# First tile of a fused attention and two-layer expert kernel: where TensorE's first value block, gate blocks and scores stand

## The chip, the core and the metric

The kernel runs on one core of one Trainium2 chip. The metric is the device time of one execution in microseconds (us), the median of the runs shown. Profiles come from one profiled execution. Engines: TensorE (PE), VectorE (DVE), ScalarE (ACT), GpSimd (POOL), and SyncE (SP), which issues transfers. The granted clock of TensorE is given in shares of its full speed: 1.00 is 2.4 GHz, 0.50 is 1.2 GHz.

## What is computed

Three stages in float32, each on 1152 rows (2 batches of 576 tokens) of 512 columns. Top-32 attention with 8 heads of 64, a gated feed-forward layer, and an expert layer with 8 experts. Cut to what matters:

```
scores = q @ k.T / sqrt(64)                       # per batch and head, 576 x 576
kth = 32nd largest of each row;  scores below kth are masked
x = softmax(scores) @ v                           # heads side by side: 1152 x 512
xn = x / sqrt(mean(x*x) + 1e-6) * rms_g
x = (silu(xn @ w_gate) * (xn @ w_val)) @ w_out    # 512 -> 1536 -> 512
e = argmax(x @ r_gate);  p = softmax(x @ r_gate)[e]
out = p * (relu(x @ w1[e]) @ w2[e])               # at most 288 rows to an expert
```

## The kernel before

**Tiles, pairs and slots.** The rows are cut into 9 tiles of 128, the heads into 4 pairs. One pair of heads of one tile is a unit of attention work; there are 36, g = 0 to 35. Every engine runs a loop over slots n. In slot n VectorE finds the top 32 of pair n (eight at a time: MAX8, L1279, L1293 and L1301, and MATCH_REPLACE, L1285 and L1297), while the other engines carry pair g = n - 1 on: GpSimd makes the bias from the thresholds (L1468, L1472), ScalarE the marks (L1003), GpSimd takes them off the scores (L1480), ScalarE makes the exponentials in place (L1013), TensorE turns them in three parts (L489 for each head of the pair, in the text "the first turn" and "the second turn", and L495 for the rest of both), ScalarE copies each part to `pt` (L868), TensorE multiplies with v (L505, "the values"), and ScalarE copies the result to `oT` (L868) at the start of the next slot. In slot n TensorE also makes the scores of pair n + 1 (L478), which ScalarE copies to `s_ring` (L868).

**The dense work.** Feed-forward work of a finished tile is laid between the attention steps. A slot has three places, ALPHA, BETA and GAMMA; tables at the head of the file say in which slot and place a piece falls, counted from the slot FIRST = 6 for tile 0. There are three gate blocks (G) and three value blocks (V) of 512 columns. For tile 0 gate block 0 falls into slot 5 BETA, value block 0 into 6 ALPHA, gate block 1 into 6 BETA, value block 1 into 7 ALPHA, gate block 2 into 7 BETA, value block 2 into 7 GAMMA. Gate blocks go to the PSUM bank `blk[1]`, value blocks to `blk[0]`. ScalarE takes tanh of a gate block (L886), VectorE finishes silu from it and the bank (L1213), ScalarE copies a value block to `xrow` (L896), and GpSimd multiplies the two into `hid` (L1417). TensorE turns `hid` (L463) and multiplies with w_out (L548).

**High and low parts.** Matrices of this layer are multiplied as the sum of three products, high x high, high x low and low x high. The weights are split in tile 0's time, in 12 pieces of two 128 x 512 copies: ScalarE makes the high part of a piece (L868, `w_parts<-w_loads`), in slots and places after the table HIGH; GpSimd subtracts it for the low part (L1409), after the table LOW. The normalized rows are split as well: ScalarE writes `x_hi` in four parts of 128 columns (L972), VectorE `x_lo` (L1221). For tile 0 the blocks behind gate block 0 run as three groups of four: L522 (high x high), L525 (low rows), L528 (low weights). Gate block 0, and all blocks of later tiles, run L535 and L536 in turn and then L539.

**The turn of the last pair.** Three pairs of a tile are turned back into rows in the slot before (L463). The fourth goes in slot 5, ALPHA: TensorE turns `oT` (L627), a filler of one matmul follows (L563, "the bridge"), ScalarE copies to `xrow` (`raw_last_pair`, which signals `col_copied`), GpSimd divides by the sum (L1421), and TensorE turns that back (L632). Then ScalarE makes the fourth part of `x_hi`.

**Order.** Each engine runs what stands in its program in that order, and waits at semaphores. On SyncE's queue the load of w_out and the rows of q for tile 2 are issued one behind the other (L369, L319). The rest of the kernel, from about 490 us, is the expert layer.

Of the kernel before, what the change touches and what calls it, by code (L numbers as in the profile page):

```python
# [34 lines left out]
FIRST = 6  # L35
# [13 lines left out]
X2, LOGITS, PICK, LEXP, RANK, SEND = 10, 11, 12, 14, 15, 16  # L49
LAST = 16  # L50
HIGH = {0: (0, GAMMA), 1: (0, GAMMA), 2: (0, GAMMA), 3: (0, GAMMA), 4: (1, GAMMA), 5: (1, GAMMA),
        6: (2, GAMMA), 7: (3, GAMMA), 8: (4, GAMMA), 9: (5, GAMMA), 10: (6, GAMMA), 11: (6, GAMMA)}
LOW = {0: (0, GAMMA), 1: (0, GAMMA), 2: (1, ALPHA), 3: (1, ALPHA), 4: (2, ALPHA), 5: (2, ALPHA),
       6: (3, ALPHA), 7: (4, ALPHA), 8: (5, ALPHA), 9: (6, ALPHA), 10: (7, ALPHA), 11: (7, BETA)}
HIGH_ORDER, LOW_ORDER = tuple(HIGH), tuple(LOW)
# [5 lines left out]
def build(nc, q, k, v, w_gate, w_val, w_out, rms_g, r_gate, w1, w2, out, capacity):  # L61
# [13 lines left out]
    NG = NT * HP  # L75
# [17 lines left out]
    with ctx:  # L93
# [146 lines left out]
        def due(n, at, k):  # L240

            t, off = divmod(n - FIRST - k // 3, HP)
            return t if k % 3 == at and off == 0 and 0 <= t < NT else None
# [176 lines left out]
        def _(pe):  # L420
# [139 lines left out]
            def bridge(count):  # L560

                for _ in range(count):
                    mm(blk[1][:, 0:384], ident[:], kT[0][:, 0, 0:384], start=True, stop=True)  # L563
# [54 lines left out]
            def turn_last_pair(n, t):  # L618


                for i in (3, 4):
                    before = due(n, ALPHA, OUT[i][0])
                    if before is not None:
                        ffn_out(before, i)
                    if i == 3:
                        pe.wait_ge(s["o_copied"], HP * (t + 1))
                        tr(last_ps, oT[:, HP - 1, :], ident[:]).then_inc(s["col_full"], 1)  # L627
                if t == 0:
                    bridge(1)
                pe.wait_ge(s["normed"], 2 * t + 2)  # L630
                pe.wait_ge(s["x_hi_set"], CD * t + CD - 1)
                tr(tb[:, (HP - 1) * P:HP * P], xrow[:, (HP - 1) * P:HP * P], ident[:]).then_inc(s["col_turned"], 1)  # L632

            def dense(n, at):


                for i in range(FB):
                    t = due(n, at, V[i])
                    if t is not None:
                        if i > 0:  # L640
                            pe.wait_ge(s["val_copied"], t * 3 + i)
                        elif t > 0:
                            pe.wait_ge(s["out_copied"], t)
                        ffn_block(t, (wv_hi, wv_lo), i, blk[0])
                t = due(n, at, HID[1])
                if t is not None:
                    turn_hidden(t, 1)
                for i in range(3):
                    t = due(n, at, OUT[i][0])
                    if t is not None:  # L650
                        if i == 0:
                            pe.wait_ge(s["wo_in"], 16)
                            pe.wait_ge(s["val_copied"], t * 3 + 3)
                        ffn_out(t, i)
                t = due(n, at, HID[2])
                if t is not None:
                    turn_hidden(t, 2)
                for i in range(FB):
                    t = due(n, at, G[i])
                    if t is not None:  # L660
                        if t * 3 + i > 0:
                            pe.wait_ge(s["silu_done"], t * 3 + i)
                        else:
                            pe.wait_ge(s["k1_copied"], KC)
                        ffn_block(t, (wg_hi, wg_lo), i, blk[1])
                t = due(n, at, LOGITS)
                if t is not None:

                    if t == NT - 1:
                        stay_awake(AWAKE[0])  # L670
                    pe.wait_ge(s["r_in"], 16)
                    pe.wait_ge(s["t_free"], use["lg", t])
                    for c in range(CD):
                        last = mm(tb[:, 0:E], dcol[:, c * P:(c + 1) * P], wr[:, c, :], start=(c == 0), stop=(c == CD - 1))
                    last.then_inc(s["t_full"], 1)
                    if t == NT - 1:
                        stay_awake(AWAKE[1])
                t = due(n, at, HID[0])
                if t is not None:
                    turn_hidden(t, 0)  # L680
                t = due(n, at, RANK)
                if t is not None:


                    pe.wait_ge(s["picked"], t + 1)
                    if t > 0:
                        pe.wait_ge(s["seen_set"], t)
                    pe.wait_ge(s["t_free"], use["rk", t])
                    mm(tb[:, 0:E], upper[:], onehot[:], start=True, stop=False)
                    mm(tb[:, 0:E], ones[:], seen[:], start=False, stop=True).then_inc(s["t_full"], 1)  # L690
# [8 lines left out]
            for n in range(SLOTS):  # L699
# [8 lines left out]
                if t is not None:  # L708
                    dense(n, ALPHA)
                    turn_last_pair(n, t)  # L710
                    if n + 1 < NG:
                        scores(n + 1)
                    dense(n, BETA)
                    if probs:
# [6 lines left out]
                else:  # L721
# [9 lines left out]
                    if 0 <= g < HP:  # L731
                        pe.wait_ge(s["k_acted"], KC - 1)
                        if g > 1:
                            pe.wait_ge(s["k1_copied"], min(2 * g - 2, KC))
                        bridge(EARLY[g > 0])
                    if probs:
                        turn_probs(g, 0)
                    if g == HP - 1:
# [2 lines left out]
                    for i in (2 * n - 4, 2 * n - 3):  # L741
                        if 0 <= i < KC:
# [3 lines left out]
                            if i >= 2:  # L746
                                pe.wait_ge(s["k1_copied"], i - 1)
                            turn_keys(1, i, blk[i % 2])
                    dense(n, BETA)
                    turn_out(n)  # L750
                    if probs:
                        turn_probs(g, 1)
# [437 lines left out]
        def _(dve):  # L1190
# [24 lines left out]
            def low_part(n, first=False):  # L1215
                t = due(n, ALPHA, XB)
                if t is not None and first == (t == 0):

                    dve.wait_ge(s["x_hi_set"], CD * (t + 1))
                    for c in range(CD):  # L1220
                        last = vec.scalar_tensor_tensor(out=x_lo[:, c * P:(c + 1) * P], in0=tb[:, c * P:(c + 1) * P], scalar=gain[:, c:c + 1],  # L1221
                                                        in1=x_hi[:, c * P:(c + 1) * P], op0=ALU.mult, op1=ALU.subtract)
                    last.then_inc(s["t_free"], 1)
# [40 lines left out]
            for n in range(SLOTS):  # L1264
# [15 lines left out]
                for a in range(2):  # L1280
# [4 lines left out]
                    vec.match_replace(w_top[:, a, :], m8[:, 2 * (n % 2) + a, 0, :], s_ring[:, n % SR, a, :], NEG).then_inc(s["top_step"], 1)  # L1285
                    if a == 0:
                        beside(n - 1, GAMMA)
                low_part(n, True)
                for i in (1, 2):
                    for a in range(2):  # L1290

                        dve.wait_ge(s["top_step"], done + 4 * i - 2 + a + 1)
                        vec.max(m8[:, 2 * (n % 2) + a, i, :], w_top[:, a, :]).then_inc(s["top_step"], 1)  # L1293
                    for a in range(2):

                        dve.wait_ge(s["top_step"], done + 4 * i + a + 1)
                        vec.match_replace(w_top[:, a, :], m8[:, 2 * (n % 2) + a, i, :], w_top[:, a, :], NEG).then_inc(s["top_step"], 1)  # L1297
                    beside(n, (ALPHA, BETA)[i - 1])
# [243 lines left out]
```

## Time and profile before

| | us |
|---|---|
| median of 3 runs | 658.88 (657.09 to 659.9) |
| the profiled execution | 659.04 |
| its span, first to last instruction | 657.2 |
| TensorE busy | 620.1 (94%), x3954 |
| VectorE busy | 411.8 (63%) |
| ScalarE busy | 327.2 (50%) |
| GpSimd busy | 264.3 (40%) |
| mean granted clock of TensorE | 0.987 |

Busy time counts overlapping parts of an engine once. Times inside the trace are counted from the start of the span. A row of a timeline may merge several instructions (x4); what stands in square brackets is the engine's idle time before it, and what ended that.

### The profile page before, as it was taken

To read this page: it belongs to the slowest core of one execution; us is meant where nothing else is said; L and a number is where in the kernel's file an instruction comes from. 1 tells how busy PE (TensorE), PEld (TensorE's weight loads), DVE (VectorE), ACT (ScalarE), POOL (GpSimd) and SP (SyncE) were. 2 spreads that over 40 slices of the span, in tenths; PEclk is the share of its full clock that TensorE was granted. 3 is DMA by queue.
4 is the path that set the end of the run, shared out by engine and by line. 5 is a ranking of instruction groups with operands and counts; after the bars stand their busy time and mean duration, and the time that the engine had idled before them with its cause. 6 is when DMAs were issued, how large, how long until landed. Compare 5 with 4: busy or idle time off the path is not lost.

```text
span 657.2 us, 11168 instructions
## 1 busy us (share of the span) xinstructions
PE 620.1 (94%) x3954; PEld 476.8 (73%) x3954; DVE 411.8 (63%) x912; ACT 327.2 (50%) x713; POOL 264.3 (40%) x366
## 2 busy tenths in 40 slices
PE   6789899999999999999999999999999999999994
PEld 5465665775775775765766766756669999999994
DVE  5999997898898897897997996921111111111110
ACT  5777766766756756756766766743210101111100
POOL 2866764555454364364454453552310100111101
PEclk9799899999999999999999999999999999999998
DMA  9999700000000000000000000000396767767501
GB/s 242 204 382 334 202 5 0 9 26 1 17 17 2 18 17 0 17 17 1 17 17 1 1 17 1 0 18 1 103 392 221 259 225 257 245 217 268 170 1 38
DMA packets 55182, 65.45 MB, mean 100 GB/s; under 512 B 32282, under 2 KB 32282, under 8 KB 55132
## 3 DMA queue, kind: packets, MB, share of 16 engines
q1 hardware_dynamic: 53388, 60.05, 28.8%
q0 software_dynamic: 1744, 4.76, 2.0%
q8 instruction: 28, 0.46, 0.3%
q14 instruction: 22, 0.18, 0.1%
HBM read 52.89 MB, written 12.30 MB: 99 GB/s over the span
## 4 chain that ended last, share of the span: by engine, by line
PE 80%; ACT 9%; POOL 6%; issue 3%; DMA 1%; SPq 0%; POOLq 0%; ACTq 0%
PE ps L809 11%; PE ps L795 11%; PE ps L548 11%; PE ps L535 7%; PE ps L539 7%; PE ps L536 7%; PE ps L505 5%; PE ps L478 5%; PE ps L489 4%; PE ps L463 3%; POOL s_ring L1480 3%; ACT pt L868 2%; PE ps L563 2%; POOL hid L1417 2%; ACT z_pair L1003 1%
## 5 line engine op out<-in xcount | busy, mean ns | idle before, releaser
L1480 POOL TENSOR_TENSOR s_ring<-s_ring,z_pair 128x576 f32<-128x576 f32 x72 | 101.0, 1425 | 71.1 <-ACT z_pair L1003 71.1
L1297 DVE MATCH_REPLACE8 w_top<-m,w_top 128x576 f32<-128x576 f32 x144 | 105.9, 744 | 0.0
L1293 DVE MAX8 m<-w_top 128x8 f32<-128x576 f32 x144 | 101.7, 748 | 0.0
L548 PE MATMUL ps<-wo_space,hid 128*128 128x512 f32 x216 | 99.3, 593 | 0.4 <-issue 0.4
L535 PE MATMUL ps<-w_parts,x_hi 128*128 128x512 f32 x196 | 81.8, 417 | 0.0
L536 PE MATMUL ps<-w_parts,x_hi 128*128 128x512 f32 x196 | 77.5, 395 | 0.0
L809 PE MATMUL ps<-arena,w_loads 128*128 128x168 f32 x512 | 75.8, 307 | 0.5 <-issue 0.5
L795 PE MATMUL ps<-arena,w_loads 128*128 128x168 f32 x512 | 74.3, 306 | 0.6 <-ACT arena L868 0.6
L1503 POOL DMA_INDIRECT out_rows<-arena,s_ring x16 | 15.1, 944 | 147.0 <-DVE arena L1321 144.6
L795 PEld LDWEIGHTS ps<-arena,w_loads 128*128 128x128 f32 x512 | 73.3, 190 | 0.9 <-ACT arena L868 0.9
L809 PEld LDWEIGHTS ps<-arena,w_loads 128*128 128x128 f32 x512 | 73.2, 190 | 0.6 <-issue 0.6
L1013 ACT ACTIVATE s_ring<-s_ring,nbias 128x576 f32<-128x576 f32 x72 | 55.8, 775 | 25.5 <-POOL s_ring L1480 25.5
L548 PEld LDWEIGHTS ps<-wo_space,hid 128*128 128x128 f32 x216 | 37.8, 190 | 34.5 <-issue 34.5
L1279 DVE MAX8 m<-s_ring 128x8 f32<-128x576 f32 x72 | 52.0, 750 | 14.2 <-ACT s_ring L868 14.2
L505 PE MATMUL ps<-pt,arena 128*64 128x128 f32 (+1 forms) x800 | 49.6, 274 | 7.1 <-ACT pt L868 7.1
L1003 ACT ACTIVATE z_pair<-s_ring,nbias 128x576 f32<-128x576 f32 x72 | 51.7, 769 | 8.9 <-POOL nbias L1468 8.9
L505 PEld LDWEIGHTS ps<-pt,arena 128*64 128x64 f32 x800 | 41.0, 141 | 19.5 <-issue 10.1
L489 PE MATMUL ps<-ident,s_ring 128*128 128x128 f32 x288 | 44.6, 277 | 9.8 <-ACT pt L868 5.5
L539 PE MATMUL ps<-w_parts,x_lo 128*128 128x512 f32 x196 | 53.7, 396 | 0.0
L1285 DVE MATCH_REPLACE8 w_top<-m,s_ring 128x576 f32<-128x576 f32 x72 | 53.3, 744 | 0.0
L868 ACT ACTIVATE pt<-ps 128x512 f32<-128x512 f32 (+1 forms) x108 | 48.9, 489 | 8.3 <-PE ps L489 8.3
L1301 DVE MAX8 m<-w_top 128x8 f32<-128x576 f32 x72 | 50.8, 748 | 0.0
(142 smaller groups left out, 887.0 us busy)
## 6 DMA issues: line engine op xcount, KB each, us to landing
w_loads<-in_moe_w SPq DMA_DIRECT2D x16, 2048.0 KB, 8.9
dispatched_rows<-drow SPq DMA_DIRECT2D x18, 260.0 KB, 8.1
w_loads<-in_moe_w_gate SPq DMA_DIRECT2D x3, 1024.0 KB, 7.2
w_loads<-in_moe_w_val SPq DMA_DIRECT2D x3, 1024.0 KB, 9.4
wo_space<-in_moe_w_out SPq DMA_DIRECT2D x1, 3072.0 KB, 12.1
arena<-dispatched_rows SPq DMA_DIRECT2D x8, 341.2 KB
out_rows<-drow SPq DMA_DIRECT2D x9, 256.0 KB, 4.9
q_space<-in_q SPq DMA_DIRECT2D x8, 256.0 KB, 3.0
```

Source lines behind the costliest of these rows:

```text
L489: last = tr(pt_ps[:, j * P:(j + 1) * P], s_ring[:, g % SR, a, a * KL + j * P:a * KL + (j + 1) * P], ident[:])
L505: last = mm(oT_ps[a * D:(a + 1) * D, r0:r1], vs[b][:, j, 2 * hp + a, :], pt[:, at + r0:at + r1], start=(j == 0), stop=(j == KC - 1))
L535: mm(bank, x_hi[:, c * P:(c + 1) * P], w_hi[:, c, :], start=(c == 0), stop=False)
L536: mm(bank, x_hi[:, c * P:(c + 1) * P], w_lo[:, c, :], start=False, stop=False)
L539: last = mm(bank, x_lo[:, c * P:(c + 1) * P], w_hi[:, c, :], start=False, stop=(c == CD - 1))
L548: last = mm(blk[0], hid[:, c * P:(c + 1) * P], wo_s[:, c, :], start=(c == 0), stop=(c == CF - 1))
L795: last = mm(ps[:, 2 + n % 2, (f % 2) * MAIN:(f % 2 + 1) * MAIN], w1_s[par][:, c, f * P:(f + 1) * P], xT[par][:, c, :], start=(c == 0), sto ...
L809: last = mm(ps[:, 4 + n, (d % 2) * MAIN:(d % 2 + 1) * MAIN], w2_s[par][:, f, d * P:(d + 1) * P], hT[:, f, :], start=(f == 0), stop=(f == C ...
L868: return nc.scalar.activation(dst, src, ACT.Copy)
L1293: vec.max(m8[:, 2 * (n % 2) + a, i, :], w_top[:, a, :]).then_inc(s["top_step"], 1)
L1297: vec.match_replace(w_top[:, a, :], m8[:, 2 * (n % 2) + a, i, :], w_top[:, a, :], NEG).then_inc(s["top_step"], 1)
L1480: gp.tensor_tensor(row, row, z_pair[:, a, :], ALU.subtract).then_inc(s["lowered"], 1)
```

## The change

Five edits, all on the first tile but for one comparison that leaves the later tiles as they are:

- TensorE: value block 0 of tile 0 runs right behind gate block 0 in slot 5 (BETA), no longer in slot 6 (ALPHA).
- TensorE: in slots 6 and 7 the work of BETA (gate blocks 1 and 2) stands ahead of both turns, no longer between them.
- TensorE: in slot 5 the scores of pair 6 stand between the bridge and the second turn of the last pair (behind a new wait for `col_copied`), no longer behind that turn.
- ScalarE: the high part of piece 8 moves from slot 4, GAMMA, to slot 5, ALPHA, between the marks and the exponentials.
- VectorE: `x_lo` of tile 0 moves behind the next two MAX8.

```diff
-        6: (2, GAMMA), 7: (3, GAMMA), 8: (4, GAMMA), 9: (5, GAMMA), 10: (6, GAMMA), 11: (6, GAMMA)}
+        6: (2, GAMMA), 7: (3, GAMMA), 8: (5, ALPHA), 9: (5, GAMMA), 10: (6, GAMMA), 11: (6, GAMMA)}
...
                 if t == 0:
                     bridge(1)
+                    pe.wait_ge(s["col_copied"], 1)
+                    scores(n + 1)
                 pe.wait_ge(s["normed"], 2 * t + 2)
...
                 for i in range(FB):
                     t = due(n, at, V[i])
-                    if t is not None:
+                    if t is not None and t + i > 0:
...
                         ffn_block(t, (wg_hi, wg_lo), i, blk[1])
+                        if t + i == 0:
+
+                            ffn_block(t, (wv_hi, wv_lo), i, blk[0])
...
                     turn_last_pair(n, t)
-                    if n + 1 < NG:
+                    if t > 0 and n + 1 < NG:
                         scores(n + 1)
...
                         bridge(EARLY[g > 0])
+                    early = n in (FIRST, FIRST + 1)
+                    if early:
+                        dense(n, BETA)
                     if probs:
                         turn_probs(g, 0)
...
-                    dense(n, BETA)
+                    if not early:
+                        dense(n, BETA)
                     turn_out(n)
...
-                low_part(n, True)
                 for i in (1, 2):
                     for a in range(2):
 
                         dve.wait_ge(s["top_step"], done + 4 * i - 2 + a + 1)
                         vec.max(m8[:, 2 * (n % 2) + a, i, :], w_top[:, a, :]).then_inc(s["top_step"], 1)
+                    if i == 1:
+                        low_part(n, True)
```

TensorE, slot 5, from the first turn of the last pair to the scores of pair 7. Before:

```order
L627 MATMUL ps<-ident,oT 128x128
L563 MATMUL ps<-arena,ident 128x384
L632 MATMUL ps<-ident,xrow 128x128
L478 MATMUL ps<-arena,q_cols 128x288 x4
...
L539 MATMUL ps<-w_parts,x_lo 128x512 x4
L489 MATMUL ps<-ident,s_ring 128x128 x8
L495 MATMUL ps<-ident,s_ring 128x128
L505 MATMUL ps<-pt,arena 64x128 x10
L522 MATMUL ps<-w_parts,x_hi 128x512 x4
L525 MATMUL ps<-w_parts,x_lo 128x512 x4
L528 MATMUL ps<-w_parts,x_hi 128x512 x4
L478 MATMUL ps<-arena,q_cols 128x288 x4
```

and now (L634 is the line that was L632):

```order
L627 MATMUL ps<-ident,oT 128x128
L563 MATMUL ps<-arena,ident 128x384
L478 MATMUL ps<-arena,q_cols 128x288 x4
L634 MATMUL ps<-ident,xrow 128x128
...
L539 MATMUL ps<-w_parts,x_lo 128x512 x4
L522 MATMUL ps<-w_parts,x_hi 128x512 x4
L525 MATMUL ps<-w_parts,x_lo 128x512 x4
L528 MATMUL ps<-w_parts,x_hi 128x512 x4
L489 MATMUL ps<-ident,s_ring 128x128 x8
L495 MATMUL ps<-ident,s_ring 128x128
L505 MATMUL ps<-pt,arena 64x128 x10
L478 MATMUL ps<-arena,q_cols 128x288 x4
```

The scores (L478) moved ahead of the last pair's second turn, and the three groups of value block 0 ahead of both turns of the probabilities (L489 x8 is both). The left-out rows are those of gate block 0.

TensorE, slot 6, from the scores of pair 7 to the values of pair 5. Before:

```order
L478 MATMUL ps<-arena,q_cols 128x288 x4
L463 MATMUL ps<-ident,q_space 128x128 x4
L489 MATMUL ps<-ident,s_ring 128x128 x4
L522 MATMUL ps<-w_parts,x_hi 128x512 x4
L525 MATMUL ps<-w_parts,x_lo 128x512 x4
L528 MATMUL ps<-w_parts,x_hi 128x512 x4
L489 MATMUL ps<-ident,s_ring 128x128 x4
L495 MATMUL ps<-ident,s_ring 128x128
L463 MATMUL ps<-ident,hid 128x128 x4
L505 MATMUL ps<-pt,arena 64x128 x10
```

and now:

```order
L478 MATMUL ps<-arena,q_cols 128x288 x4
L463 MATMUL ps<-ident,q_space 128x128 x4
L522 MATMUL ps<-w_parts,x_hi 128x512 x4
L525 MATMUL ps<-w_parts,x_lo 128x512 x4
L528 MATMUL ps<-w_parts,x_hi 128x512 x4
L489 MATMUL ps<-ident,s_ring 128x128 x8
L495 MATMUL ps<-ident,s_ring 128x128
L463 MATMUL ps<-ident,hid 128x128 x4
L505 MATMUL ps<-pt,arena 64x128 x10
```

Gate block 1 stood between the two turns and now stands ahead of both. In slot 7 gate block 2 moves in the same way.

ScalarE, end of slot 4 to the first exponential of slot 5. Before:

```order
L868 ACTIVATE arena<-ps 128x4x64
L868 ACTIVATE w_parts<-w_loads 128x512 x2
L868 ACTIVATE oT<-ps 128x128
L868 ACTIVATE xrow<-ps 128x128
L972 ACTIVATE x_hi<-ps,gain 128x128 x4
L977 ACTIVATE hid,ssq<-xrow 128x512
L1003 ACTIVATE z_pair<-s_ring,nbias 128x576 x2
L1013 ACTIVATE s_ring,den<-s_ring,nbias 128x576
```

and now (each line number is 9 higher):

```order
L877 ACTIVATE arena<-ps 128x4x64
L877 ACTIVATE oT<-ps 128x128
L877 ACTIVATE xrow<-ps 128x128
L981 ACTIVATE x_hi<-ps,gain 128x128 x4
L986 ACTIVATE hid,ssq<-xrow 128x512
L1012 ACTIVATE z_pair<-s_ring,nbias 128x576 x2
L877 ACTIVATE w_parts<-w_loads 128x512 x2
L1022 ACTIVATE s_ring,den<-s_ring,nbias 128x576
```

The two copies of piece 8 (`w_parts<-w_loads`) moved from ahead of the `oT` copy to behind the marks.

## Rows read from the trace of the kernel before

**Rows 1.** Windows of TensorE: stretch, length, busy us (instructions), granted clock, DMA share, GB/s.

```profile
60.00:98.00 38.00, 33.12 (x200) 0.96 0.49 130
115.00:450.00 335.00, 325.50 (x2078) 1.00 0.04 11
```

**Rows 2.** Timeline of TensorE, slot 5: start, us, engine, line, operation, count, idle before.

```profile
60.36 0.33 PE L627 MATMUL ps<-ident,oT 128*128 128x128 f32 x1 [0.56 <-ACT oT L868]
...
61.92 0.30 PE L632 MATMUL ps<-ident,xrow 128*128 128x128 f32 x1 [0.59 <-ACT x_hi L972]
62.15 1.24 PE L478 MATMUL ps<-arena,q_cols 64*128 64x288 f32 x8
63.32 0.50 PE L535 MATMUL ps<-w_parts,x_hi 128*128 128x512 f32 x1
...
66.38 0.66 PE L489 MATMUL ps<-ident,s_ring 128*128 128x128 f32 x4
68.89 0.63 PE L489 MATMUL ps<-ident,s_ring 128*128 128x128 f32 x4 [1.86 <-ACT pt L868]
...
70.37 2.24 PE L505 MATMUL ps<-pt,arena 128*64 128x128 f32 x20 [0.74 <-ACT pt L868]
72.54 1.85 PE L522 MATMUL ps<-w_parts,x_hi 128*128 128x512 f32 x4
...
76.19 1.24 PE L478 MATMUL ps<-arena,q_cols 64*128 64x288 f32 x8
```

**Rows 3.** Windows of TensorE again, shorter stretches with idle time in them.

```profile
12.00:16.00 4.00, 2.59 (x18) 1.00 1.13 349
...
43.00:48.00 5.00, 4.52 (x27) 1.00 1.06 382
...
70.50:71.00 0.50, 0.50 (x8) 0.59 1.31 237
```

**Rows 4.** Timeline of ScalarE, end of slot 4 to slot 6.

```profile
58.96 1.18 ACT L868 ACTIVATE w_parts<-w_loads 128x512 fp32r<-128x512 f32 x2
...
65.46 0.78 ACT L1013 ACTIVATE s_ring<-s_ring,nbias 128x576 f32<-128x576 f32 x1 [0.89 <-POOL s_ring L1480]
...
68.16 0.58 ACT L868 ACTIVATE pt<-ps 128x512 f32<-128x512 f32 x1
...
72.68 0.28 ACT L868 ACTIVATE oT<-ps 128x128 f32<-128x128 f32 x1 [0.74 <-PE ps L505]
...
76.29 0.69 ACT L896 ACTIVATE xrow<-ps,rinv 128x512 f32<-128x512 f32 x1 [0.25 <-PE ps L528]
77.50 0.65 ACT L868 ACTIVATE s_ring<-ps 128x576 f32<-128x576 f32 x1 [0.52 <-PE ps L478]
...
79.82 0.61 ACT L868 ACTIVATE pt<-ps 128x512 f32<-128x512 f32 x1
81.28 0.69 ACT L886 ACTIVATE hid<-ps,rinv 128x512 f32<-128x512 f32 x1 [0.86 <-PE ps L528]
```

**Rows 5.** Timeline of GpSimd, slot 7.

```profile
86.10 2.81 POOL L1480 TENSOR_TENSOR s_ring<-s_ring,z_pair 128x576 f32<-128x576 f32 x2 [4.60 <-ACT z_pair L1003]
```

**Rows 6.** Timeline of TensorE, slots 6 and 7.

```profile
78.21 1.18 PE L522 MATMUL ps<-w_parts,x_hi 128*128 128x512 f32 x4
...
81.08 0.60 PE L489 MATMUL ps<-ident,s_ring 128*128 128x128 f32 x4
...
82.68 1.31 PE L505 MATMUL ps<-pt,arena 128*64 128x128 f32 x20 [0.45 <-ACT pt L868]
...
94.92 1.20 PE L528 MATMUL ps<-w_parts,x_hi 128*128 128x512 f32 x4 [0.56 <-POOL w_parts L1409]
```

**Rows 7.** Timeline of VectorE, slot 5.

```profile
62.66 1.13 DVE L1221 SCALAR_TENSOR_TENSOR x_lo<-ps,gain,x_hi 128x128 fp32r<-128x128 f32 x4 [1.59 <-ACT x_hi L972]
```

**Rows 8.** SyncE's queue at 59.57, and the landing times of loads into q_space.

```profile
59.57 0.91 SPq L319 DMA_DIRECT2D q_space<-in_q  x1
...
DMA to landing us min/median/max: 2.8/3.0/12.9
```

More of the change, by code:

```diff
@@ L638, in dense @@
                     t = due(n, at, V[i])
-                    if t is not None:
+                    if t is not None and t + i > 0:
                         if i > 0:
                             pe.wait_ge(s["val_copied"], t * 3 + i)
-                        elif t > 0:
+                        else:
                             pe.wait_ge(s["out_copied"], t)
```

## Prediction, made before the changed kernel was run

> **What bounds the kernel now.** I read the windows by stage first. TensorE is busy 325.50 of 335.00 us between 115 and 450, but only 33.12 of 38.00 us between 60 and 98, at a mean granted clock of 0.96 [rows 1]. So the long middle is TensorE's own work in program order, and time can only be won where TensorE waits before it: slots 5 to 7, the first tile. Whatever TensorE is ahead by at the end of slot 7 should be kept to the end, since nothing after it is tied to a fixed time.
>
> In slot 5 [rows 2] the reader is to see three losses: 0.56 us before L627; 1.86 us between the two turns of the probabilities (L489), and 0.74 us before the values (L505); and then the clock. It is granted in full up to 70.5 and is then at half (1.2 GHz) [rows 3], so that L505 takes 2.24 us where it takes 1.31 in the next slot, and the L522 of the value block 1.85 against 1.18 [rows 2, 6]. In slot 7 TensorE waits once more, 0.56 us, for the low part of a weight piece from GpSimd (L1409), before the third group of value block 2, at 94.92 [rows 6]. That wait is the one that ends last in this stage: before it GpSimd is released only at 86.10, after 4.60 us of idle time for ScalarE's marks [rows 5].
>
> **Part 1, piece 8's high copies move from slot 4 to slot 5.** On ScalarE they stood before the copy to oT: 1.18 us for two, or 1.04 in a row with others [rows 4]. The 0.56 us that TensorE waited for oT go, and 0.1 of overlap with it: L627 at 59.71 instead of 60.36, 0.65 earlier. In slot 5 the copies stand between marks and exponentials, where ScalarE waited 0.89 us for GpSimd [rows 4]; the marks come 0.15 earlier, so 1.04 lies in a hole of 0.89 + 0.15. I price it at nothing; without that cover it costs 1.0 of ScalarE.
>
> **Part 2, scores ahead of the last pair's second turn.** They take 1.17 us (62.15 to 63.32), and fill the time in which TensorE waited 0.59 us for x_hi before L632 [rows 2]. From L627 to the gate block were 63.32 - 60.36 = 2.96; without the 0.59 and the bridge's small overlap it is 2.3, and 59.71 + 2.3 = 62.0: 1.3 us earlier, 0.65 of it from part 1. The added wait is for ScalarE's copy behind L627, which is done while the bridge runs; it costs nothing, and is bounded by the 0.59 that it replaces. Behind it on TensorE stands everything, so if that copy came late all would.
>
> **Part 3, VectorE.** It stood 1.59 us for x_hi before x_lo [rows 7]; now two MAX8 (1.3 us) come first. VectorE gains about 1.4, and x_lo is ready by 63.6, before the gate block's eight high matmuls end at 64.0. So nothing new waits. VectorE's gain is of no use here: its thresholds are ready before ScalarE and GpSimd take them up.
>
> **Part 4, value block 0 behind gate block 0.** Gate 3.06 us (63.32 to 66.38), value 2.87 at full clock (78.21 to 81.08) [rows 2, 6]: from 62.0 TensorE is busy to 67.95. The first turn follows at once, ends at 68.55 (0.6 long, as at 81.08 [rows 6]), and ScalarE copies it at 68.62 instead of 68.16 [rows 4]. From that copy to the second turn are 0.73 us and from there to the values 1.48 (68.16, 68.89, 70.37) [rows 2, 4], so the values start at 70.83, 0.46 late. Of 1.86 + 0.74 us of idle time 0.8 + 0.74 stay. I take the clock as full there: 1.25 for the values instead of 2.17 gives 72.08 against 72.54. ScalarE has its own copies in front until 72.32, so oT goes from 72.68 to 72.32, 0.36 us earlier. That is all that the critical chain has won by here, although scores of pair 7 on TensorE are now at 72.7 instead of 76.19 [rows 2]: TensorE has gained 3.5 us, of which nearly all is value block 0, taken out of its way.
>
> **Part 5, slot 6.** ScalarE's chain starts 0.36 earlier. On it lay two waits for TensorE, 0.25 us before the value copy and 0.52 before the score copy [rows 4]; both go, with 0.2 us of overlap lost at them. So the copy of the first turn, at 79.82 [rows 4], comes at 79.82 - 0.36 - 0.97 = 78.5. TensorE had the gate block between the turns; now it stands before them, from 74.4 (scores and the turn of q take 1.7 after 72.7) to 77.2, and TensorE idles from 77.8 to the second turn at 78.5 + 0.73 = 79.2. This 1.4 us is the wait that replaces the old ones. Behind the copy ScalarE waited 0.86 us for the gate block [rows 4]; that goes too, 0.2 to 0.3 of it comes back as a wait for the second turn. 1.33 + 0.86 - 0.2 = 2.0 us: the hidden copy, the four weight copies and oT of slot 7 come 2.0 earlier.
>
> One load is moved nearer to its use. The rows of q for tile 2 are issued at 59.57, and the longest landing of that tile is 12.9 us [rows 8]: 72.5. The turn is now at 73.9, a margin of 1.4; I price it at nothing. If it landed w later than 73.9, the idle time before the second turn would cover 0.7 of it.
>
> Gate block 1 now also stands earlier behind its wait for silu 0. That follows ScalarE's tanh right behind the copies of slot 5 and one operation of VectorE, so by about 72; the margin is 2 us, and gate block 2 has 3 or more in slot 7. I price both at nothing.
>
> **Part 6, slot 7.** Marks, and with them GpSimd's run from 86.10, come 2.0 earlier, at 84.1. GpSimd works without a pause from there to the low part of piece 11, so this ends at 92.9 instead of 94.9, and the third group of value block 2 starts there instead of at 94.92 [rows 5, 6]. TensorE by its own path: values at 80.67, value block 1 and scores to 86.1, gate block 2 to 88.96, second turn 90.35 after a hole of 0.9 (0.73 behind the copy again), value block 2 from 90.9, its third group two thirds of 2.87 behind, at 92.9. The two paths meet within 0.1, so **both must be early for the gain to be 2.0 us**.
>
> **Sum.** 0.36 + 0.97 + 0.66 = 2.0. Profiled execution: 659.04 - 2.0 = 657.0; its span 657.2 becomes 655.2. The median of the runs shown, 658.88, stands 0.16 under it, which gives 656.9. The bounds: below, if every wait in slots 5 to 7 went and the clock stayed full, 0.56 + 0.59 + 1.86 + 0.74 + 0.56 and 0.93 + 0.67 of clock, 5.9 us; above, the rival on the clock.
>
> **Rival 1, the clock falls in slot 6.** The half clock in slot 5 came after idle times of 1.86 and 0.74 us close together. In the stretch 12 to 16, with 2.59 us busy of 4 and one idle time of 1.4 us, it did not fall [rows 3]. My new hole in slot 6 is 1.4 us with 0.3 more behind it, nearer to the second row. If it falls, L505 and L522 pay 0.93 + 0.67 = 1.6 us on TensorE's path, which has no slack: gain 0.4, 658.5. The page "TensorE: Matmul & The Clock Gate" of the Trainium skill says ("HAM oscillation") that idle gaps over about 3 us are to be avoided; by it neither hole would count, but the trace disagrees, for the longest idle time before the fall here was 1.86.
>
> **Rival 2, the clock falls in slot 5 all the same.** After 67.95 come only turns, with holes of 0.8 and 0.74, until 70.8. The values then take 0.93 more, oT comes at 73.2, and ScalarE's chain with it: 2.0 - 0.9 = 1.1 gained, 657.8. Against it: in 43 to 48, which holds the same kind of turns around one hole of 0.74, the clock stayed at 1.00 [rows 3]. The same page of the Trainium skill (Part 4, PE-mode transpose) says that transposes do not count as busy like matmuls; by that rule this rival is the likely one. The row at 43 to 48 leans against it, but bridges stand in that stretch too.
>
> **Rival 3, more than the sum.** If ScalarE's copies fit the holes better than I place them, TensorE could keep more of the 3.5 us that it is ahead by at 72.7. GpSimd's run from 86.10 speaks against it. It would give 3.5 to 4.5: 654.9.
>
> **Rival 4, slower.** Both falls of the clock together. ScalarE's chain loses 0.9 in slot 5, and TensorE 1.6 behind the hole of slot 6: 2.0 - 0.9 - 1.6 = -0.5, so 659.4. It decides from the point at which the second hole (1.4 us) is enough; the full clock at 12 to 16 speaks against it.
>
> **How the numbers follow.** Forecast 656.9: 0.58. Rival 1: 0.13. Rival 2: 0.12. Rival 3: 0.11. Rival 4: 0.06. The runs shown lie 2.8 us apart, so a median of a few runs can stand 1 us off; the forecast's own range is 655.6 to 658.2. For 8 in 10 I take in rivals 1 and 2: 655.0 to 659.2. What a measurement of this kernel can tell from no change is about 0.5%, 3.3 us. Only rival 3, most of it, and a tail of the forecast lie beyond it on the fast side: 0.14. On the slow side a tail of rival 4: 0.03. Within it: 0.83.
>
> **What the profile after would show.** Right: L627 at 59.7 and the gate block at 62.0; the second turn of slot 5 near 69.3; scores of pair 7 near 72.7; a hole of 1.4 us before the second turn of slot 6; GpSimd's run of slot 7 from 84.1; the third group of value block 2 at 92.9; clock 1.00 from 60 to 98. Wrong: the clock at 0.50 anywhere in 70 to 85 (rivals 1, 2 and 4); TensorE waiting for q; a shift at 92.9 that is not found again at 450, which would mean that the middle is not tied to TensorE alone.

## The result, and the profile after

| | before | changed |
|---|---|---|
| median | 659.06 us (6 runs, 657.09 to 659.9) | 656.82 us (6 runs, 656.08 to 656.89) |
| profiled execution, its span | 659.04, 657.2 | 656.66, 654.7 |
| TensorE busy | 620.1 | 618.9 |
| mean granted clock | 0.987 | 0.991 |

The ratio is 0.9967, with a 95% interval of 0.9953 to 0.9981: 0.3% faster, clear of no change by its interval, though less than the 0.5% that the prediction took for the least that a measurement can tell. 656.9 was forecast. The three runs shown with the prediction had a median of 658.88; with three more it is 659.06.

TensorE's windows after, to be laid beside [rows 1] and [rows 3] (stretch, length, busy us, granted clock, DMA share, GB/s):

```profile
60.00:98.00 38.00, 33.51 (x205) 1.00 0.48 131
115.00:450.00 335.00, 325.52 (x2075) 1.00 0.04 11
```

```profile
66.00:78.00 12.00, 9.34 (x65) 1.00 0.96 243
76.83:80.31 3.48, 1.85 (x14) 1.00 0.27 61
```

The long middle is as busy as it was (325.52 of 335 against 325.50). The clock is full throughout 60 to 98, where its mean was 0.96. TensorE's timeline of slots 5 to 7 after, which answers to [rows 2] and [rows 6]:

```profile
59.68 0.33 PE L627 MATMUL ps<-ident,oT 128*128 128x128 f32 x1
...
60.59 1.24 PE L478 MATMUL ps<-arena,q_cols 64*128 64x288 f32 x8
61.76 0.33 PE L634 MATMUL ps<-ident,xrow 128*128 128x128 f32 x1
61.85 0.48 PE L535 MATMUL ps<-w_parts,x_hi 128*128 128x512 f32 x1
...
64.84 1.09 PE L522 MATMUL ps<-w_parts,x_hi 128*128 128x512 f32 x4
...
67.64 0.60 PE L489 MATMUL ps<-ident,s_ring 128*128 128x128 f32 x4
69.02 0.63 PE L489 MATMUL ps<-ident,s_ring 128*128 128x128 f32 x4 [0.78 <-ACT pt L877]
...
70.50 1.31 PE L505 MATMUL ps<-pt,arena 128*64 128x128 f32 x20 [0.75 <-ACT pt L877]
72.37 1.24 PE L478 MATMUL ps<-arena,q_cols 64*128 64x288 f32 x8 [0.56 <-ACT oT L877]
...
78.83 0.63 PE L489 MATMUL ps<-ident,s_ring 128*128 128x128 f32 x4 [1.40 <-ACT pt L877]
...
89.99 0.63 PE L489 MATMUL ps<-ident,s_ring 128*128 128x128 f32 x4 [0.78 <-ACT pt L877]
90.49 1.18 PE L522 MATMUL ps<-w_parts,x_hi 128*128 128x512 f32 x4
...
92.55 1.21 PE L528 MATMUL ps<-w_parts,x_hi 128*128 128x512 f32 x4
```

L627 waits no more; the scores stand ahead of L634 and fill its wait; value block 0 (L522 at 64.84) stands ahead of the first turn, which comes later for it, so that only 0.78 of the wait of 1.86 us behind that turn is left; L505 takes 1.31 us, not 2.24. New waits are 0.56 us before the scores of pair 7 (L478) and 1.40 us before the second turn of slot 6. The third group of value block 2 starts at 92.55 instead of 94.92, 2.37 us earlier. That shift goes on unchanged: the last L627 stands at 445.96 (448.40 before), and the first matmul of the expert loop at 487.16 (489.59 before), 2.43 earlier.

```profile
445.96 0.27 PE L627 MATMUL ps<-ident,oT 128*128 128x128 f32 x1
```

```profile
487.16 9.36 PE L804 MATMUL ps<-arena,w_loads 128*128 128x168 f32 x64 [0.65 <-ACT arena L877]
```

ScalarE and GpSimd after, beside [rows 4] and [rows 5]:

```profile
68.27 0.60 ACT L877 ACTIVATE pt<-ps 128x512 f32<-128x512 f32 x1
...
71.94 0.29 ACT L877 ACTIVATE oT<-ps 128x128 f32<-128x128 f32 x1
...
78.07 0.61 ACT L877 ACTIVATE pt<-ps 128x512 f32<-128x512 f32 x1
```

```profile
83.74 2.81 POOL L1490 TENSOR_TENSOR s_ring<-s_ring,z_pair 128x576 f32<-128x576 f32 x2 [3.59 <-ACT z_pair L1012]
...
90.10 2.39 POOL L1419 TENSOR_TENSOR w_parts<-w_loads,w_parts 128x1024 fp32r<-128x1024 f32 x1
```

### The profile page after: what moved, and what is told of

It is laid out like the page before. It is cut to its first block, busy times and chain, and to the rows that moved or that the text cites. A ratio compares the mean times of both kernels' runs of the same rounds, so it can differ in the third digit from the quotient of the medians.

```text
span 654.7 us, 11169 instructions
## 1 busy us (share of the span) xinstructions
PE 618.9 (95%) x3954; PEld 476.5 (73%) x3954; DVE 411.6 (63%) x912; ACT 327.0 (50%) x713; POOL 264.0 (40%) x366
## 4 chain that ended last, share of the span: by engine, by line
PE 82%; ACT 8%; POOL 5%; issue 3%; POOLq 0%; ACTq 0%
PE ps L818 11%; PE ps L804 11%; PE ps L548 11%; PE ps L535 7%; PE ps L539 7%; PE ps L536 7%; PE ps L505 5%; PE ps L478 5%; PE ps L489 5%; PE ps L463 3%; POOL s_ring L1490 2%; ACT pt L877 2%; PE ps L563 2%; POOL hid L1427 2%; ACT z_pair L1012 1%
## 5 line engine op out<-in xcount | busy, mean ns | idle before, releaser
L1301 DVE MAX8 m<-w_top 128x8 f32<-128x576 f32 x144 | 101.5, 746 | 0.0
L505 PE MATMUL ps<-pt,arena 128*64 128x128 f32 (+1 forms) x800 | 48.6, 271 | 6.8 <-ACT pt L877 6.8
L489 PE MATMUL ps<-ident,s_ring 128*128 128x128 f32 x288 | 45.0, 279 | 10.5 <-ACT pt L877 6.6
L505 PEld LDWEIGHTS ps<-pt,arena 128*64 128x64 f32 x800 | 40.3, 139 | 19.4 <-issue 10.1
L539 PE MATMUL ps<-w_parts,x_lo 128*128 128x512 f32 x196 | 53.9, 396 | 0.0
L489 PEld LDWEIGHTS ps<-ident,s_ring 128*128 128x128 f32 x288 | 33.3, 142 | 24.9 <-issue 10.8
```

Source lines behind the costliest of these rows:

```text
L489: last = tr(pt_ps[:, j * P:(j + 1) * P], s_ring[:, g % SR, a, a * KL + j * P:a * KL + (j + 1) * P], ident[:])
L505: last = mm(oT_ps[a * D:(a + 1) * D, r0:r1], vs[b][:, j, 2 * hp + a, :], pt[:, at + r0:at + r1], start=(j == 0), stop=(j == KC - 1))
L539: last = mm(bank, x_lo[:, c * P:(c + 1) * P], w_hi[:, c, :], start=False, stop=(c == CD - 1))
```

## How the experiments are read

The start of the kernel (the same in all kernels here, up to the values of pair 3 in slot 4) is not equally long in every execution: these values (L505) start between 56.48 and 58.51 in the traces below, and single executions of one kernel lie up to 4 us apart. A part of that is the clock, which also falls in slot 1. There TensorE's waits are nearly the same in all traces (1.37 to 1.96 us, 1.28 to 1.30 and 0.73 to 0.84), but the clock does not behave the same behind them. Before, and e7:

```profile
23.63 0.66 PE L489 MATMUL ps<-ident,s_ring 128*128 128x128 f32 x4 [1.51 <-ACT s_ring L1013]
25.58 0.63 PE L489 MATMUL ps<-ident,s_ring 128*128 128x128 f32 x4 [1.29 <-ACT pt L868]
...
27.15 2.40 PE L505 MATMUL ps<-pt,arena 128*64 128x128 f32 x20 [0.84 <-ACT pt L868]
```

```profile
24.06 0.66 PE L489 MATMUL ps<-ident,s_ring 128*128 128x128 f32 x4 [1.37 <-ACT s_ring L1022]
26.00 0.63 PE L489 MATMUL ps<-ident,s_ring 128*128 128x128 f32 x4 [1.28 <-ACT pt L877]
...
27.58 1.31 PE L505 MATMUL ps<-pt,arena 128*64 128x128 f32 x20 [0.84 <-ACT pt L877]
```

The mean clock from 24 to 36 is 0.72 in nine of the fourteen traces (before and changed among them), 0.86 in e1, e4, e9 and e12, and 1.00 in e7 alone. From 36 to 646 it is 1.00 in all traces but that of the kernel before, where it is 0.86 from 66 to 78.

So beside the median each run (e1 to e12, told below) is read by two distances within its own trace: **D**, from the start of the values of pair 3 to the third group of value block 2 (L528, slot 7), and **F**, from the first turn of slot 5 (L489) to that group. Kernel before: D = 94.92 - 57.96 = 36.96, F = 94.92 - 66.38 = 28.54. Changed: D = 92.55 - 57.97 = 34.58, F = 92.55 - 67.64 = 24.91. D fell by 2.38. F counts value block 0 only where it stands behind the first turn, so it compares like with like only. Differences of 0.1 us in D are near what one trace can tell; one source of them is named under e10.

| run | edit | D | F | median |
|---|---|---|---|---|
| before | | 36.96 | 28.54 | 659.06 |
| changed | | 34.58 | 24.91 | 656.82 |
| e1 | before + five fillers | 35.92 | 27.51 | 658.75 |
| e9 | before + two fillers | 35.37 | 26.96 | 657.94 |
| e2 | before + value block 0 | 35.98 | 24.90 | 658.18 |
| e3 | changed, gate blocks back | 34.47 | 24.90 | 656.52 |
| e4 | changed, start of slot 5 back | 35.98 | 24.92 | 657.98 |
| e11 | changed, piece 8 back | 35.18 | 24.92 | 656.60 |
| e10 | changed, VectorE back | 34.47 | 24.90 | 656.42 |
| e5 | changed, piece 11 late | 34.36 | 24.80 | 656.35 |
| e6 | changed, q copy behind | 34.45 | 24.88 | 656.45 |
| e7 | piece 11 late, gate blocks back | 35.21 | 23.93 | 655.45 |
| e8 | e7 + q copy behind | 33.47 | 23.86 | 655.51 |
| e12 | e7 + VectorE back | 33.52 | 23.95 | 655.14 |

Runs e1 to e4 shared runs of the kernel before with a median of 659.33, e5 to e8 of 659.28, e9 to e11 of 660.00, e12 of 660.29.

## Was it the clock? Fillers in the old kernel

e1 and e9 leave all work where it was and only keep TensorE busy in the hole of 1.86 us.

```diff
+            def fill(count):
+                for _ in range(count):
+                    mm(blk[0][:, 0:384], ident[:], kT[0][:, 0, 0:384], start=True, stop=True)
...
                         turn_probs(g, 0)
+                    if t == 0:
+                        fill(4)            # e9: fill(2)
                     turn_out(n)
                     if probs:
                         turn_probs(g, 1)
                         turn_rest(g)
+                    if t == 0:
+                        fill(1)            # e9: none
```

> The kernel before, with five filler matmuls (128x384, 0.37 us each) in slot 5: four in the hole of 1.86 us between the two turns, one in the hole of 0.74 us before the values. Nothing useful is moved. Theory (the clock carries most of the gain): the clock stays at 1.00 between 66 and 77, the values take 1.31 instead of 2.24 us and the value block 1 us less, the oT copy comes at 71.9 instead of 72.7, and the third group of value block 2 at 93.3 instead of 94.9: 1.6 us faster than before, so 657.5. Rival (the moved work itself is what gains): the holes are as long as before, so within 0.3 us of before, 659.0.

Measured: 658.75, ratio 0.9988 (0.9971 to 1.0004). The clock stayed at 1.00 from 66 to 78, but F fell by 1.03 only, from 28.54 to 27.51 (D by 1.04). The fillers were mis-sized: one issued matmul of this form is two records of 0.37 us each, so four of them lasted from 66.06 to 68.64. The distance from the scores of slot 5 to the second turn grew from 6.74 to 68.64 - 61.34 = 7.30, 0.56 late.

```profile
61.34 1.24 PE L478 MATMUL ps<-arena,q_cols 64*128 64x288 f32 x8
...
66.06 2.75 PE L567 MATMUL ps<-arena,ident 128*128 128x384 f32 x8
68.64 0.60 PE L489 MATMUL ps<-ident,s_ring 128*128 128x128 f32 x4
```

> The kernel before, with two filler matmuls (0.74 us each, as the bridge shows: 0.81 for its two records) in the hole of 1.86 us between the two turns of slot 5, and none before the values. The run with five was mis-sized: its four took 2.6 us and made the second turn 0.56 late. Theory (the half clock is 1.6 of the gain, and the fall comes from this hole): nothing is late, the clock stays at 1.00 from 66 to 78, the third group of value block 2 is 1.5 us nearer to the first turn of slot 5 (28.54 us before): 27.0. Median 657.5, and no execution at the low end of the mean clocks that the kernel before shows (0.986). Rival (fillers don't replace the moved work): 28.5 us, and a median of 659.

```profile
65.19 0.66 PE L489 MATMUL ps<-ident,s_ring 128*128 128x128 f32 x4
65.68 1.46 PE L567 MATMUL ps<-arena,ident 128*128 128x384 f32 x4
67.69 0.63 PE L489 MATMUL ps<-ident,s_ring 128*128 128x128 f32 x4 [0.56 <-ACT pt L874]
...
69.18 1.31 PE L505 MATMUL ps<-pt,arena 128*64 128x128 f32 x20 [0.75 <-ACT pt L874]
...
92.15 1.20 PE L528 MATMUL ps<-w_parts,x_hi 128*128 128x512 f32 x4 [0.59 <-POOL w_parts L1415]
```

Measured: F = 26.96 against 27.0 foretold, D 1.59 shorter than before. The values take 1.31 us again and nothing is late. Median 657.94 against 660.00, ratio 0.9983 (0.9969 to 0.9996). The mean clocks of its twelve executions are 0.990 to 0.993; those of the kernel before beside them are 0.986 to 0.993, with 22 of 26 at or under 0.988. So filling one hole with useless work is worth 1.6 us: **in the kernel before, keeping the clock up gains by itself two thirds of what the whole change gains**. The hole of 1.86 us was needed for that fall: with 0.56 and 0.75 us left in its place, none is in the trace. That it is enough is not shown, as slot 1 ends both ways behind the same waits. Nor does a run tell how much of the 2.4 us the changed kernel would lose if its clock fell in slot 5 all the same; that its work also moved makes the two numbers different questions.

## What each part is worth

```diff
 e2, against the kernel before
-                    if t is not None:
+                    if t is not None and t + i > 0:
...
                         ffn_block(t, (wg_hi, wg_lo), i, blk[1])
+                        if t + i == 0:
+                            ffn_block(t, (wv_hi, wv_lo), i, blk[0])

 e3, against the changed kernel
-                    early = n in (FIRST, FIRST + 1)
+                    early = False

 e4, against the changed kernel
-        6: (2, GAMMA), 7: (3, GAMMA), 8: (5, ALPHA), ...
+        6: (2, GAMMA), 7: (3, GAMMA), 8: (4, GAMMA), ...
...
-                    pe.wait_ge(s["col_copied"], 1)
-                    scores(n + 1)
...
-                    if t > 0 and n + 1 < NG:
+                    if n + 1 < NG:
                         scores(n + 1)

 e11, against the changed kernel: the first two lines of e4 alone

 e10, against the changed kernel
+                low_part(n, True)
                 for i in (1, 2):
...
-                    if i == 1:
-                        low_part(n, True)
```

> The kernel before, with value block 0 behind gate block 0 and nothing else of the change. Theory (ScalarE's chain and TensorE's path both count): the gate block starts at 63.3 as before, the first turn at 69.2, the values at 72.05 at full clock, the oT copy 0.9 late at 73.6; in slot 6 ScalarE's two waits for TensorE (0.25 and 0.52) go, and the second turn comes at 80.1 instead of 81.1: 1.0 us faster than before, 658.1. Rival (the clock is all): 1.6 us faster, since the clock is full here too, 657.5. Rival (this part is the whole change): 2.4 us faster, as the full change.

Measured: D 0.98 shorter, foretold 1.0. The second turn of slot 6 stands 80.76 - 58.50 = 22.26 behind the values of pair 3, before 81.08 - 57.96 = 23.12. Median 658.18, ratio 0.9985 (0.9965 to 1.0005). The clock was full, and yet it gained 0.6 less than the fillers of e9. The block stands ahead of the first turn, which comes 2.66 later behind the values of pair 3 (69.58 - 58.50 against 66.38 - 57.96), and ScalarE's oT copy comes 15.38 behind them, where it came 14.72 behind before and comes 13.84 behind in e9.

> The changed kernel, with gate blocks 1 and 2 put back between the turns. Theory: in slot 6 TensorE idles 1.3 us before the first turn instead of 1.4 before the second, and the second turn comes at 78.8 as in the changed kernel; in slot 7 TensorE gains 0.5, but waits for GpSimd's low part of piece 11 at 92.5. Same time as the changed kernel within 0.2 us, 656.8. Rival (the early gate blocks carry part of the gain): 1 us slower than the changed kernel, 657.8. Rival (the hole of 1.3 us close behind those of slot 5 lets the clock fall): 1.0 to 1.6 us slower than the changed kernel.

Measured: D 0.11 shorter than the changed kernel's, median 656.52. The hole has only changed its place, from before the second turn to before the first:

```profile
75.60 0.66 PE L489 MATMUL ps<-ident,s_ring 128*128 128x128 f32 x4 [1.14 <-ACT s_ring L1022]
...
92.80 1.19 PE L528 MATMUL ps<-w_parts,x_hi 128*128 128x512 f32 x4 [0.60 <-POOL w_parts L1419]
```

The edit of the gate blocks is worth nothing here (F 24.90 against 24.91). Without it TensorE comes 0.60 us too early to GpSimd's low part in slot 7 instead of arriving together with it.

> The changed kernel without its two edits at the start of slot 5: piece 8 copied in slot 4 again, and the scores of pair 6 behind the second turn of the last pair. Theory: the gate block starts at 63.3 instead of 61.85, everything on ScalarE's chain in slot 5 is 1.5 later, and the gain over before falls from 2.4 to 0.8: 658.3. Rival (the start of slot 5 is hidden behind ScalarE's own work): within 0.3 us of the changed kernel, 657.0.

Measured: D 1.40 longer than the changed kernel's, foretold 1.5 (the 0.8 against before came out as 0.98). Median 657.98. D is that of e2 to the hundredth, though the two kernels differ by the gate blocks and VectorE's edit; those two are worth nothing together in that trace.

> The changed kernel, with piece 8's high copies back in slot 4, and the scores still ahead of the last pair's second turn. Theory (part 1 of the prediction): L627 waits 0.56 us again, ScalarE has 1.04 less to do between marks and exponentials, and the first turn of slot 5 comes 0.65 later; 0.6 us slower than the changed kernel, 657.4. Rival (ScalarE's copy of the first turn is late for its own work, so TensorE's 0.65 is hidden): within 0.2 us of the changed kernel, 656.8.

Measured: D 0.60 longer than the changed kernel's, as foretold. L627 waits its 0.56 us again. The median, 656.60, does not show it (the changed kernel's is 656.82) and by itself would fit the rival. The trace shows it.

```profile
60.86 0.33 PE L627 MATMUL ps<-ident,oT 128*128 128x128 f32 x1 [0.56 <-ACT oT L877]
```

> The changed kernel, with VectorE's x_lo back ahead of the two MAX8. Theory (VectorE's gain is of no use, part 3 of the prediction): the same as the changed kernel within 0.2 us, 656.8. Rival (VectorE's thresholds are late without it, since pair 5's are then ready at 70.6 and pair 6's at 80.9, close to where GpSimd takes them up): 0.3 to 1.3 us slower, 657.1 to 658.1.

Measured: D 0.11 shorter than the changed kernel's, median 656.42. GpSimd waits 1.59 us for the thresholds of pair 6 (0.27 in the changed kernel) and then 2.25 instead of 3.59 for ScalarE's marks, so they come in time. The edit gains nothing, in this trace, and perhaps costs the 0.1: from L634 to value block 0 are 3.08 us in the changed kernel and 2.98 here. But 2.98 is found in e3, e5, e6 and e11 as well, which have the edit, so VectorE is only just in time with it. More on it below.

The parts in this order: value block 0 0.98, piece 8 0.60, scores ahead of the second turn 1.40 - 0.60 = 0.80, gate blocks and VectorE 0, together 2.38. That they add up to what D fell by is no test: they are differences between neighbouring kernels, and e2 and e4 happen to have the same D. Against e10, whose D is 34.47, piece 8 would come out as 0.7.

## Do two paths meet at the end of slot 7?

```diff
 e5, against the changed kernel (piece 11's high copies late)
-        ... 10: (6, GAMMA), 11: (6, GAMMA)}
+        ... 10: (6, GAMMA), 11: (7, ALPHA)}

 e6, against the changed kernel, on ScalarE
-                    if next_tile(n) is not None:
+                    if next_tile(n) is not None and n != FIRST:
                         q_columns(next_tile(n))
                     if here:
                         turned_probs(g, 0)
+                    if n == FIRST:
+                        q_columns(next_tile(n))

 e7 = e5 and e3;  e8 = e5, e3 and e6;  e12 = e5, e3 and e10
```

> The changed kernel, with ScalarE's two high copies of piece 11 moved from the end of slot 6 behind the marks of slot 7. They stood ahead of the marks that release GpSimd. Theory (two paths meet): GpSimd's run of slot 7 starts 1.0 us earlier, but TensorE's own path reaches the third group of value block 2 at 92.4 instead of 92.55: 0.1 us faster than the changed kernel, 656.7. Rival (GpSimd's run alone sets the end of slot 7): 1.0 us faster, 655.8.

Measured: GpSimd's run starts at 82.47, 15.08 behind the first turn of slot 5; in the changed kernel 83.74 - 67.64 = 16.10. So it is 1.02 earlier, and the third group only 0.11 (F 24.80 against 24.91). The rival's 1.0 did not come. Median 656.35.

> The changed kernel, with ScalarE's q copy of slot 6 (0.47 us) behind the copy of the first turn instead of ahead of it. Theory (two paths meet, and both hang on this copy): the hole of 1.40 us before the second turn of slot 6 shrinks to 0.9, and both paths are 0.4 earlier at 92.5: 0.4 us faster than the changed kernel, 656.4. Rival (the hole is harmless): no change.

The hole shrank as foretold, from 1.40 to 0.90, but F fell by 0.03 only, and TensorE has a wait for GpSimd where it had none:

```profile
78.71 0.63 PE L489 MATMUL ps<-ident,s_ring 128*128 128x128 f32 x4 [0.90 <-ACT pt L877]
...
92.91 1.20 PE L528 MATMUL ps<-w_parts,x_hi 128*128 128x512 f32 x4 [0.23 <-POOL w_parts L1421]
```

That two paths meet is right, that both hang on this copy is wrong. ScalarE does the same work in another order; it loses a wait of 0.23 us for the turn and gets one of 0.21 for the next (L463). GpSimd's run starts 84.08 - 68.03 = 16.05 behind the first turn, as late as before. Median 656.45.

> The changed kernel, with piece 11 late as in the run of that name, and gate blocks 1 and 2 between the turns again. Theory: now both paths of slot 7 are shortened, GpSimd's by 1.0 and TensorE's by 0.5, so the third group comes 0.5 earlier, 656.3. Rival (one of the two paths alone counts): 1.0 us or 0.0 faster than the changed kernel.

F fell by 0.98, to 23.93, not by 0.5. Both edits alone gave 0.11 or less. Mis-sized was TensorE's own path: besides the 0.5 us, the 0.32 us that it waited for the exponentials at the first turn of slot 7 (in e3) went too, since they come earlier when two copies less stand before the marks, and about 0.1 of waiting for GpSimd at the group itself. Median 655.45 (655.28 to 655.82), ratio 0.9945 (0.9927 to 0.9963). This run also showed something that no theory had, told below.

> The changed kernel, with piece 11 late, the q copy behind the first turn's copy, and gate blocks 1 and 2 between the turns. Theory: TensorE's path gains 0.5 in slot 7 and 0.2 in slot 6: 0.7 us faster than the changed kernel, 656.1. Rival (the hole at the first turn lets the clock fall): slower than the changed kernel.

F 23.86, 0.07 less than in e7, where 0.2 was foretold: the q copy is worth little here as well. The clock did not fall. Median 655.51.

## Where VectorE's edit costs

In the trace of e7 the clock never fell before slot 5, and TensorE was 1.5 us ahead there:

```profile
12.00:45.00 33.00, 26.79 (x158) 1.00 1.14 312
```

```profile
58.19 0.33 PE L627 MATMUL ps<-ident,oT 128*128 128x128 f32 x1
...
63.93 1.20 PE L539 MATMUL ps<-w_parts,x_lo 128*128 128x512 f32 x4 [1.46 <-DVE x_lo L1230]
```

```profile
61.44 1.41 DVE L1301 MAX8 m<-w_top 128x8 f32<-128x576 f32 x2
62.77 1.11 DVE L1230 SCALAR_TENSOR_TENSOR x_lo<-ps,gain,x_hi 128x128 fp32r<-128x128 f32 x4
```

VectorE did not wait for x_hi at all; it had its two MAX8 to do first, and TensorE stood 1.46 us before the low rows, so that all it had been ahead by was lost. D is 35.21 there. In e8, which has the same edit on VectorE, TensorE is late (L627 at 59.86), doesn't wait, and D is 33.47.

> The kernel of the run with piece 11 late and the gate blocks between the turns, and in addition VectorE's x_lo ahead of the two MAX8 again, as in the kernel before. In that run TensorE was 1.5 us ahead at slot 5 and waited 1.46 us for x_lo, since VectorE, which had not waited for x_hi at all, made its two MAX8 first. Theory (the edit on VectorE costs time whenever TensorE comes early): a median of 655.0 against 655.45, executions down to 652.6 + 1.8 = 654.4 or less, and no wait over 0.3 us before L539 in slot 5. Where TensorE isn't early, the same as that run. Rival (VectorE's thresholds bind instead): no execution under 655.2, the least of that run was 655.28.

```profile
58.33 0.33 PE L627 MATMUL ps<-ident,oT 128*128 128x128 f32 x1
...
62.43 1.11 PE L539 MATMUL ps<-w_parts,x_lo 128*128 128x512 f32 x4
...
90.13 1.19 PE L528 MATMUL ps<-w_parts,x_hi 128*128 128x512 f32 x4
```

```profile
61.17 1.13 DVE L1230 SCALAR_TENSOR_TENSOR x_lo<-ps,gain,x_hi 128x128 fp32r<-128x128 f32 x4 [0.24 <-ACT x_hi L981]
```

TensorE is as early (L627 at 58.33), and there is no wait before L539. D is 33.52 instead of 35.21, and the span of the profiled execution 652.5, the shortest of all. Median 655.14 (5 runs, 654.44 to 656.11), ratio 0.9933 (0.992 to 0.9947). The least execution, 654.44, misses the bound of 654.4 by 0.04 and lies below the rival's 655.2. The median is 0.3 below that of e7, on another chip, which the spread of either does not tell from nothing; the missing wait in the trace does.

e12 is 0.7% faster than the kernel before. Against the changed kernel its D is 1.06 shorter and its F 0.96, and its interval (0.992 to 0.9947) lies below that of the changed one (0.9953 to 0.9981). The two were not run side by side, and the runs of the kernel before beside them differ (660.29 and 659.06), so the traces are the better witness. It keeps value block 0, the scores and piece 8 of the change, takes its other two edits back, and moves piece 11's high copies behind the marks of slot 7.

## Why the prediction was right

The mechanism was right, and its terms were small by 0.4 us in all. That 656.9 was met within 0.1 us is in part luck: in the trace the gain was 2.4 us and not 2.0, and the median of the kernel before rose by 0.18 with three more runs.

- **What bounds it.** Right. The shift at 92.55 (2.37) is found again at 446 (2.44) and at 487 (2.43).
- **Parts 1 and 2.** L627 at 59.68 (59.71 foretold), the gate block at 61.85 (62.0). Piece 8's copies on ScalarE cost nothing behind the marks. Measured apart, the two parts are 0.60 and 0.80 (e11, e4), where the sum had 0.65 for each.
- **Part 3.** In the profiled execution right within 0.1 us: VectorE's edit gains nothing (e10). But "nothing new waits" holds only where TensorE is no earlier than in that trace. In e7 the edit cost 1.46 us. The prediction had one trace of the start and took its times as given.
- **Part 4.** Second turn 69.02 (69.35), values 70.50 (70.83), oT copy 71.94 (72.32), hole 0.78 (0.8), clock full. The 0.35 us by which all was early is the mis-sized term: gate and value block ran in 67.64 - 61.85 = 5.79 us where the sum had 5.93, and the gate block began 0.15 sooner. It is also most of why the gain was 2.4 and not 2.0.
- **Part 5.** The copy of the first turn at 78.07 (78.5), the new hole 1.40 us (1.4), the second turn at 78.83 (79.2). Right in kind and size. The load of q's rows was in time: the turn follows the scores without a wait.
- **Part 6.** GpSimd from 83.74 (84.1), its last low part ends at 90.10 + 2.39 = 92.49, TensorE's own path would have been at 90.49 + 1.94 = 92.43 (1.94 is what the two groups before take in e7, where nothing waits), and the group starts at 92.55. That both had to be early is shown by e5 (one alone: 0.11) and e7 (both: 0.98).
- **The clock.** Rivals 1, 2 and 4 did not come: 1.00 throughout. The Trainium skill ("TensorE: Matmul & The Clock Gate", Part 4, PE-mode transpose) says that a transpose does not count as PE-busy in the way that a matmul does, and the prediction put it on the side of rival 2. The traces here don't decide on that. The stretch 76.83 to 80.31 of the changed kernel holds turns alone, 1.85 us busy of 3.48, and the clock stayed at 1.00 in it and behind it; it also stayed in e7 through 22.69 to 27.58, turns alone, 1.40 us busy of 4.89. But behind or within that same stretch of slot 1 it fell in the other thirteen traces, and in the kernel before it fell behind 66.38 to 70.37, turns alone, 1.39 us busy of 3.99.
- **What the sum did not say.** It gave the clock about 0.9 us, in one term, and then let the chain take it over. e9 shows that in the kernel before the clock alone is worth 1.6 us. The total was right, but a reader of the sum would have taken the moved work for nearly the whole cause, and would not have seen that two filler matmuls reach two thirds of the gain.
- **Rival 3** did not come with this change; e12, whose D is 3.44 shorter than before's, shows how it could: by shortening both paths at once.

## What to carry to other kernels

A hole on TensorE can cost more than its own length: behind the one of 1.86 us the half clock cost 1.6 us more in later matmuls. Before moving useful work into a hole, fill it with a matmul that writes to a free bank: two lines tell what the clock alone is worth. Look at the granted clock of every early stretch in every trace, since a fall can come in one execution and not in the next (slot 1 here), and compare distances within a trace. Where two chains meet at one wait, an edit that shortens one of them measures as nothing and is still half of the gain, so try such edits in pairs. And work put ahead of something that "waits anyway" is a cost in the executions in which it doesn't wait.

## What the runs showed of the hardware

- In slots 5 to 7 the clock fell behind idle times of 1.86 and 0.74 us close together, and not behind 0.56 + 0.75 (e9), 0.78 + 0.75 + 0.56 (changed) or 1.40 (changed), nor in a stretch of 3.48 us with 1.85 us of turns. In slot 1 it fell behind 1.51 + 1.29 + 0.84 (before) and behind 1.37 + 1.28 + 0.84 (e9), and did not behind the same 1.37 + 1.28 + 0.84 in e7. So the lengths of the waits alone don't settle it; what does is open.
- The mean clock of an execution tells how much of it ran at half clock, not where. e2 (0.990) and e4 (0.993) both had a full clock in slot 5 and differ in slot 1 (0.72 and 0.86 from 24 to 36). Beside e9 to e11, the kernel before has spans of 655.5 to 655.9 at 0.993, one of 656.0 at 0.990, 657.1 to 657.6 at 0.988 (one 659.0), 658.1 to 658.9 at 0.986, and at 0.987 in between 657.2 to 658.4. The short ones can be executions without the fall of slot 5, without that of slot 1, or with less of it; no trace of one was taken, so this stays open. In an execution of the kernel before in which the clock doesn't fall in slot 5, the change would gain about 0.8 us, an estimate from D in e9 and in the changed kernel (35.37 - 34.58).
- One issued float32 matmul of 128 x 384 is two records, 0.81 us in all for one, 1.46 for two.
